# A fused attention and MLP kernel: outputs of 15 attention chunks computed with channels on partitions and turned to rows by DMA, and three moves in the order of the side work

## The reference

```
state = alpha[t, :, None] * state + k[t] (outer) v[t]
y[t]  = q[t] @ state
```

## Time and profile before

| | |
|---|---|
| median of 3 runs | 753.81 us (753.63 to 753.96) |
| the profiled execution | 753.43 us, span in the profile 751.9 us |
| PE busy | 741.3 us, 99% of the span |
| DVE, ACT, POOL busy | 457.1, 300.3, 60.0 us |
| granted PE clock | full speed in all 40 slices |
| chain that ended last | PE 89%, DVE 5%, DMA 2%, ACT 2% |

### The profile page before, as it was taken

How to read it: one execution, slowest core, us unless ns; L and a number is a source line. 1 busy time by engine, 2 the same in 40 slices (tenths; PEclk the granted TensorE clock), 3 DMA queues, 4 the chain that set the end, 5 groups by cost and what they waited for, 6 DMA issues and landing times.

```text
span 751.9 us, 16930 instructions
## 1 busy us (share of the span) xinstructions
PE 741.3 (99%) x6898; PEld 717.1 (95%) x6898; DVE 457.1 (61%) x1056; ACT 300.3 (40%) x517; POOL 60.0 (8%) x124
## 2 busy tenths in 40 slices
PE   8999999999999999999999999999999999999998
PEld 7889989899999899999999999999999999999998
DVE  7887777957677477774786764247443664243322
ACT  3453232626544364463543344143522434141511
POOL 1100000000000000000005000200021000200000
PEclk9999999999999999999999999999999999999999
DMA  8362214273533536335344421040103101010100
GB/s 246 113 172 82 72 43 135 58 175 82 152 77 78 143 104 115 103 112 153 80 137 132 147 48 52 3 135 32 33 32 120 49 16 47 0 35 28 39 25 32
DMA packets 77809, 64.64 MB, mean 86 GB/s; under 512 B 44788, under 2 KB 72680, under 8 KB 77736
## 3 DMA queue, kind: packets, MB, share of 16 engines
q1 hardware_dynamic: 77736, 63.62, 31.7%
HBM read 43.65 MB, written 13.37 MB: 76 GB/s over the span
## 4 chain that ended last, share of the span: by engine, by line
PE 89%; DVE 5%; DMA 2%; ACT 2%; issue 1%; POOL 0%; DVEq 0%; POOLq 0%; ACTq 0%
PE h L125 14%; PE h L127 12%; PE h L126 12%; PE acc L125 12%; PE acc L127 12%; PE acc L126 12%; PE side_bank L1691 2%; DMA kT_planes<-k_planes 2%; PE side_bank L126 2%; PE side_bank L127 2%; PE side_bank L1704 2%; PE side_bank L125 2%; PE side_bank L1622 1%; PE side_bank L1634 1%; DVE F_inv L1146 1%
## 5 line engine op out<-in xcount | busy, mean ns | idle before, releaser
L194 ACT ACTIVATE hT_high<-h 128x384 fp32r<-128x384 f32 (+1 forms) x204 | 96.1, 471 | 319.6 <-PE h L127 319.4
L199 DVE SCALAR_TENSOR_TENSOR hT_low<-h,hT_high 128x384 fp32r<-128x384 f32 (+1 forms) x204 | 108.3, 531 | 172.3 <-ACT hT_high L194 171.3
L125 PE MATMUL h<-xnT_high,w_high 128*128 128x384 f32 (+1 forms) x612 | 207.0, 338 | 0.9 <-DVE w_low L258 0.9
L127 PE MATMUL h<-xnT_high,w_low 128*128 128x384 f32 (+1 forms) x612 | 199.3, 326 | 0.0
L126 PE MATMUL h<-xnT_low,w_high 128*128 128x384 f32 (+1 forms) x612 | 199.2, 325 | 0.0
L125 PE MATMUL acc<-w_high,hT_high 128*128 128x384 f32 x576 | 193.6, 336 | 0.5 <-DVE hT_low L199 0.5
L127 PE MATMUL acc<-w_high,hT_low 128*128 128x384 f32 x576 | 192.8, 335 | 0.0
L126 PE MATMUL acc<-w_low,hT_high 128*128 128x384 f32 x576 | 192.5, 334 | 0.0
L125 PEld LDWEIGHTS h<-xnT_high,w_high 128*128 128x128 f32 x612 | 115.1, 188 | 5.0 <-DVE w_low L258 1.0
L126 PEld LDWEIGHTS h<-xnT_low,w_high 128*128 128x128 f32 x612 | 115.3, 188 | 0.0
L127 PEld LDWEIGHTS h<-xnT_high,w_low 128*128 128x128 f32 x612 | 115.1, 188 | 0.0
(11 more groups left out here) (152 smaller groups left out, 801.0 us busy)
## 6 DMA issues: line engine op xcount, KB each, us to landing
stage<-w_dram SPq DMA_DIRECT2D x24, 384.0 KB, 3.6
x_scratch<-x_unit SPq DMA_DIRECT2D x8, 576.0 KB, 3.6
a_in<-alpha_dram SPq DMA_DIRECT2D x6, 672.0 KB, 4.9
q_in<-q_dram SPq DMA_DIRECT2D x6, 672.0 KB, 6.5
k_in<-k_dram SPq DMA_DIRECT2D x6, 672.0 KB, 8.5
v_in<-v_dram SPq DMA_DIRECT2D x6, 576.0 KB, 3.7
xb<-x_scratch SPq DMA_DIRECT2D x4, 576.0 KB, 4.3
xb<-x_turned SPq DMA_DIRECT2D x4, 576.0 KB, 7.0
```

Of the source, the lines that this page charges most:

```text
L125: pe.matmul(out, wh, xh, start=start, stop=False)
L127: return pe.matmul(out, wl, xh, start=False, stop=stop)
L194: act.activation(self.hT[0][:, j % H_SLOTS, 0:u.cols], self.hps[j % H_BANKS][:, 0:u.cols], ACT.Relu).then_inc(self.h_high, 1)
L199: dve.scalar_tensor_tensor(out=self.hT[1][:, j % H_SLOTS, 0:u.cols], in0=self.hps[j % H_BANKS][:, 0:u.cols], scalar=0.0, in1=self.hT[0][:, ...
```

## The change

The outputs of the 15 REGULAR chunks are computed the other way round. Within the halves `v_in` (48 columns) is stationary and `probs` (64 columns) moving; for the carried part `state` (48 columns) is stationary and `q_mul` (64) moving. The result has channels on partitions; the first half of the tokens goes to `bank[BSC]`, the second to `bank[BY]`, and both parts are summed in place, so `copy_y` and `add_odd` go. ACT splits the result into planes (`split_y`, two ACTIVATEs), SP turns them by DMA (`turn_y`), ACT joins them to rows of x (`join_y`, two ACTIVATEs on 64 partitions each). `u_summed` is now given by the outputs within, behind the increments.

Order: chunk 2's increments and outputs (slots 6, 7) go ahead of `pe_down`. On ACT the range checks move from slots 2 and 3 to 0 and 1, `copy_kT` of chunk 2 from 6 to 5, `split_x` from 8 to 9; `join_x` and the high parts are done for two chunks in slot 10 and for the third in slot 11. On DVE `prepare_q` of the following unit moves from 6 to 7, ahead of the statistics of chunks 0 and 1; chunk 2's statistics come in slot 8 behind `prepare_k`, its normalisation in slot 9. On SP the load of alpha stands first and `load_k` ahead of `turn_k` of chunk 2; `turn_y(ONE[-1], 2)` stands behind `load_rows(0)`.

```diff
         self.next_slot, self.next_k_slot, self.next_q_slot = 6, 8, 10
+        self.ahead = ()
...
         self.rows_slot, self.range_slot = 9, 3
-        self.k_turned = self.x_turned = False
+        self.k_turned = self.x_turned = self.y_turned = False
...
 for u in REGULAR:
-    u.k_turned = u.x_turned = True
+    u.k_turned = u.x_turned = u.y_turned = True
...
     u.x_before, u.units_before = REGULAR[0].base, REGULAR[0].n
-    u.scores, u.increments, u.outputs = (0, 3, 5), (1, 4, 6), (2, 5, 7)
+    u.scores, u.increments, u.outputs, u.ahead = (0, 3, 5), (1, 4, 6), (2, 5, 7), (5, 6, 7)
...
             kT_planes = sb1("kT_planes", [P, 2 * PAIRS, R], U16)
+            y_planes = sb1("y_planes", [R, 2 * PAIRS * P], U16)
+            yT_planes = sb1("yT_planes", [P, 2 * PAIRS, 2 * ODD], U16)
...
         JOINS = {10: (0, 1), 11: (2,)}
+        FRONT, LAST = slice(0, 2 * P), slice(2 * P, UN)
...
             return (bank[BSC], m.hps[1] if u.first() else bank[BY])[two]
+        def yT_bank(i):
+            return (bank[BSC][:, 0:PAIRS * SUB], bank[BY][:, PAIRS * SUB:2 * PAIRS * SUB])[i]
...
                 sp.dma_start(v_in[:, s, :], v[0, :, g, :]).then_inc(first_v[g], 16)
-            def load_qa(u):
-                chunks = slice(u.c0, u.c0 + UT)
+            def load_a(u):
...
                 sp.wait_ge(range_checked, u.n)
-                sp.dma_start(a_in[:, :, :], aT[u.b, :, chunks, :]).then_inc(a_loaded, 16)
+                sp.dma_start(a_in[:, :, :], aT[u.b, :, u.c0:u.c0 + UT, :]).then_inc(a_loaded, 16)
+            def load_q(u):
...
                 sp.wait_ge(q_ready, u.base)
-                sp.dma_start(q_in[:, :, :], qT[u.b, :, chunks, :]).then_inc(q_loaded, 16)
+                sp.dma_start(q_in[:, :, :], qT[u.b, :, u.c0:u.c0 + UT, :]).then_inc(q_loaded, 16)
...
                 sp.dma_start_transpose(kT_planes[:, :, :], k_planes[:, :]).then_inc(kT_turned, 16)
-            def turn_x(u):
-                for c in range(UT):
+            def turn_y(u, c):
+                sp.wait_ge(y_split, u.base + c - FIRST_TURNED + 1)
+                sp.wait_ge(x_ready, u.base + c)
+                sp.dma_start_transpose(yT_planes[:, :, 0:R], y_planes[:, :]).then_inc(y_turned, 16)
+            def turn_x(u, chunks=range(UT)):
+                for c in chunks:
...
                 attending = ONE[u.n - 1]
-                turn_k(attending, 1)
-                load_qa(u)
-                turn_k(attending, 2)
+                load_a(u)
+                if attending in REGULAR:
+                    turn_k(attending, 1)
+                    turn_y(attending, 0)
+                load_q(u)
...
                 load_k(u)
+                if attending in REGULAR:
+                    turn_k(attending, 2)
+                    turn_y(attending, 1)
...
                     turn_rows(*AFTER_K[u.n])
+                if attending in REGULAR:
+                    turn_y(attending, 2)
...
                 load_v(u)
-                if attending.x_turned:
+                if attending in REGULAR:
...
             turn_k(ONE[-1], 1)
+            turn_y(ONE[-1], 0)
...
             turn_k(ONE[-1], 2)
-            turn_rows(2, 1)
+            turn_y(ONE[-1], 1)
...
             load_rows(0)
+            turn_y(ONE[-1], 2)
...
             turn_x(ONE[-1])
+            turn_rows(2, 1)
...
                 wait_apart(x_ready, u.base + u.size)
-                wait_apart(x_odd, u.base + u.size)
+                if not u.y_turned:
+                    wait_apart(x_odd, u.base + u.size)
...
                 inv_std(u, slice(0, u.size))
-            with pool.Fori(1, B) as b:
+            for u in ONE[3:5]:
+                final_rows(u)
+                inv_std(u, slice(0, 2))
+                inv_std(u, slice(2, UT))
+            with pool.Fori(2, B) as b:
...
                     u = Unit(2 * b + half + 1, b, UT * half, UT, half)
+                    u.y_turned = True
...
                                ACT.Copy).then_inc(x_joined, 1)
+            def split_y(u, c):
+                act.wait_ge(y_summed, u.base + c + 1)
+                for i in range(2):
+                    op = act.activation(y_planes[:, :].rearrange("p (w h i t) -> p w h i t", w=2, h=PAIRS, i=2)[:, :, :, i, :],
+                                        yT_bank(i)[0:R, :].bitcast(U16).rearrange("p (h t w) -> p w h t", h=PAIRS, w=2),
+                                        ACT.Copy)
+                op.then_inc(y_split, 1)
+            def join_y(u, c):
+                act.wait_ge(y_turned, 16 * (u.base + c - FIRST_TURNED + 1))
+                if c == 0 or u.slot(c) == 0:
+                    act.wait_ge(stored[u.half(c)], 16 + 16 * u.b)
+                to = x_rows(u)(c).bitcast(U16).rearrange("p (h two d w) -> p w h two d", w=2, two=2, d=D)
+                for i, sub in enumerate(SUBS):
+                    src = yT_planes[sub, :, :].rearrange("p (w h) (two d) -> p w h two d", w=2, two=2)
+                    op = act.activation(to[sub, :, :, :, :], src[:, :, :, ::(1, -1)[i], 0:D], ACT.Copy)
+                op.then_inc(x_ready, 1)
...
                 act.activation(m.xnT[u.par][0][:, k, 0:u.cols], xT_rows(u, k), ACT.Copy, scale=scale).then_inc(xT_high, 1)
+            def high_part(u, k, cols):
+                act.wait_ge(x_joined, u.base - u.x_before + cols.stop // P)
+                act.activation(m.xnT[u.par][0][:, k, cols], xT_over(u)[:, k, cols], ACT.Copy,
...
             def side_regular(u, following, slot):
                 if slot == 0:
                     copy_kT(u, 0)
+                    check_above(u)
+                if slot == 1:
+                    check_below(u)
...
                     split_k(u, 1)
-                    check_above(u)
-                    copy_y(u, 0)
+                    split_y(u, 0)
...
                     copy_kT(u, 1)
-                    check_below(u)
...
                     split_k(u, 2)
+                    join_y(u, 0)
...
                 if slot == 5:
-                    copy_y(u, 1)
+                    split_y(u, 1)
+                    copy_kT(u, 2)
...
                 if slot == 6:
-                    copy_kT(u, 2)
+                    join_y(u, 1)
...
                 if slot == 7:
-                    copy_y(u, 2)
+                    split_y(u, 2)
...
                 if slot == 8:
+                    join_y(u, 2)
+                if slot == 9:
...
                 if slot == 10:
-                    for c in range(UT):
-                        join_x(u, c)
+                    join_x(u, 0)
+                    join_x(u, 1)
+                    for k in range(KD):
+                        high_part(u, k, FRONT)
...
                 if slot == 11:
+                    join_x(u, 2)
...
                     for k in range(KD):
-                        high_xT(u, k, g_col[:, k:k + 1])
+                        high_part(u, k, LAST)
...
             dve.memset(zeros[:, :], 0.0).then_inc(zeros_done, 1)
+            dve.memset(yT_bank(1), 0.0)
...
                                              op0=ALU.mult, op1=ALU.subtract).then_inc(m.xnT_ready, 1)
+            def low_part(u, k, cols):
+                if cols == FRONT:
...
+                else:
+                    dve.wait_ge(xT_high, KD * u.n + k + 1)
+                out_, high = (part[:, k, cols] for part in reversed(m.xnT[u.par]))
+                op = dve.scalar_tensor_tensor(out=out_, in0=xT_over(u)[:, k, cols], scalar=g_col[:, k:k + 1], in1=high,
+                                              op0=ALU.mult, op1=ALU.subtract)
+                if cols == LAST:
+                    op.then_inc(m.xnT_ready, 1)
...
                     dve.wait_ge(x_ready, u.base + i + 1)
-                    dve.wait_ge(x_odd, u.base + i + 1)
+                    if not u.y_turned:
+                        dve.wait_ge(x_odd, u.base + i + 1)
...
         @block.vector
...
             def side_regular(u, following, slot):
...
                 if slot == 2:
                     prepare_q(u, 2)
-                    add_odd(u, 0)
...
                 if slot == 5:
-                    add_odd(u, 1)
...
                 if slot == 6:
+                    next_state(u, 2)
...
                         bound_alpha(following)
-                    next_state(u, 2)
+                if slot == 7:
...
                         prepare_q(following, 0)
-                if slot == 7:
-                    add_odd(u, 2)
-                    final_statistics(u)
+                    final_statistics(u, (0, 1))
...
                 if slot == 8:
-                    normalise(u, x_rows(u), xn_one)
+                    normalise(u, x_rows(u), xn_one, (0, 1))
...
                         prepare_k(following, 0)
+                    final_statistics(u, (2,))
+                if slot == 9:
+                    normalise(u, x_rows(u), xn_one, (2,))
...
                 if slot == 11:
-                    for k in range(KD):
-                        low_xT(u, k, g_col[:, k:k + 1])
```

(55 more changed lines are left out.)

11 lines of the change are left out of this document (8 added, 3 removed).

## The result

The changed kernel took 763.12 us (median of 4 runs, 761.95 to 764.38) against 753.74 us: ratio 1.0124 [1.0107 to 1.0142], 9.4 us slower. The forecast was 759.3 in a range up to 764.5, so the sign and the range held, and the size fell 3.8 us short.

What follows compares the result with a forecast made beforehand. PE, busy 741.3 of 751.9 us, was taken as the bound. New waits of 7.5 + 5.3 + 3.3, less 8.9 and 1.9, gave +5.3 us: 758.7 on the profiled execution, forecast as 759.3, range 747 to 764.5.

Steps and rivals of the forecast that it cites:

- case A: The forecast itself: three new waits outweigh PE's shorter stream, 759.3 us, own range 755.5 to 763; chance 0.62.
- PE's own gain: Side work of 15 chunks: turned outputs within and carried run faster, 0.59 us a chunk, 8.9 us in all.
- old waits that go: PE's existing waits in the hosts, for copied kT and once for the state, should vanish: 1.9 us.
- first wait: Outputs carried of chunk 0, slot 2: check_above ahead of relu(1) delays the state, 7.5 us over five hosts.
- second wait: Unit's end, pe_down(11): longer DVE and ACT chain makes the low part late, 1.3 us in four hosts, 5.3 in all.
- third wait: Increments of chunk 0, slot 1: late split_k delays kT, 0.8 us in four hosts, 3.3 us in all.
- Within 0.54: Turned outputs within take 0.54 us a chunk, saving 0.50, bounds 0.42 to 0.53.
- Carried saves 0.09: Turned outputs carried save 0.09 us a chunk, bounds 0 to 0.10.
- estimate of 11 us more: By the skill's 25 ns rule, within saves 0.13 a chunk, carried loses 0.30, some 11 us worse; prediction sided with the trace.
- The 15 more transposes sit in SP's idle time; each 1.25 us of issue: DMA queue in the hosts: the added transposes fit where SP idles, 1.25 us of issue each, and cost nothing.
- Rival F: kT of chunk 2 lands late behind the load of k, holding slot 6's increments 1.7 us a host: 767; chance 0.04.
- Costs nothing behind the hosts: Last host: turn_y of chunk 2 behind load_rows(0) lands some 1 us late, and pe_up(11) has cover for that.

Runs made afterwards that it cites:

- e1: Changed kernel with check_above put back one slot on ACT, from slot 0 to slot 1, behind relu(1): 758.36 us.
- e7: Kernel before with only the two range checks moved early, to slots 0 and 1 of ACT: 755.87 us.
- e3: Changed kernel with split_k of the following unit moved ahead of split_x of chunk 2 on ACT: 757.70 us.
- e9: Changed kernel with the row copies of batches 1 and 2 taken out of the hosts and issued later in bursts: 768.65 us.
- e5: Changed kernel with check_above behind relu(1), chunk 2's statistics ahead of prepare_k, split_k in slot 9 and one batch 1 row copy later: 758.83 us.
- e11: Changed kernel with check_above behind relu(1), chunk 2's statistics ahead of prepare_k, split_k in slot 9 and row copies issued singly: 750.61 us.

## Why the prediction was right in sign and short in size

The forecast was case A: PE's own stream gets shorter, three waits take more than that back. It named the waits by place and releaser, and all three are there, in the hosts it said. Term by term:

| term of the forecast | forecast | measured |
|---|---|---|
| PE's own gain, 15 chunks | -8.9 | -7.4 |
| old waits that go | -1.9 | -1.0 |
| first wait (outputs carried, chunk 0) | +7.5 | +6.8 |
| second wait (`pe_down(11)`) | +5.3 | +2.9 |
| third wait (kT, slot 1) | +3.3 | +3.1 |
| kT in other slots, n = 5 and 6 | 0 | +2.4 |
| lower clock in n = 5 | 0 | +1.5 |
| pipeline restarts behind waits and the rest | 0 | +0.7 |
| behind and ahead of the hosts | 0 | +1.8 |
| sum, against the span | +5.3 | +10.7 |

- **PE's gain.** "Within 0.54" was 0.56, by records that start every 17.5 ns on average. "Carried saves 0.09" failed: it saves 0.01 to 0.02. The step took the pace to be set by the stationary side, because scores (64 and 64 columns) and carried (64 and 48) ran alike. The turned carried outputs have 48 and 64 and run alike too, so 64 columns on either side go with the slower pace; the increments are the only block with 48 on both. The step also said that the turned form has a bank for each row half. That is so within the halves, but the turned carried outputs write both row halves into either bank, and no run separates the two reasons. The Trainium skill (TensorE: Matmul & The Clock Gate, section "Wait — 56ns, not 53.3ns?") says that starts are never closer than about 25 ns. Counted by records, as the prediction counted, the trace disagrees: the increments' 32 records still take 0.40 us, 12.5 ns each, and the turned 0.56 for 32 is below 25 ns too. Counted by matmuls of the program, two records each, they are 25 and 35 ns apart on average (in pairs closer, as the last section shows), and the rule would not have forbidden the gain; the estimate of 11 us more hung on the count by records.
- **Old waits.** I had worked out 1.9 from the weight loads less the entry gap; by the matmuls' own idle time there were 1.0 to take.
- **First wait.** Right, mechanism and size; e1 takes it away in four hosts and leaves 1.0 in the first, e7 makes it alone.
- **Second wait.** The count holds within 0.4 us at every point. From the end of `pe_up(7)` (212.19) the pair is normalised after 6.8 us (forecast 6.9), `prepare_k` done after 9.4 (9.5), x of chunk 2 normalised after 11.65 (12.0), `split_x` after 12.5 (12.8), relu(11) starts after 16.1 (16.5), the low part is there after 17.1 (17.5), and PE wanted it after 16.4 (16.3). But the wait is a difference of two numbers of 16 to 17 us: 0.4 less in the chain, near half of it POOL's single 1/std, 0.95 from chunk 2's statistics (222.41) to the normalisation (223.36) where I took a pair's 1.1, and 0.1 more cover made 0.7 of 1.3. The mechanism is right; the term was mis-sized by that.
- **Third wait.** Right, and e3 shows it to be worth more than its own line, because the late copy also stood ahead of the check.
- **"The 15 more transposes sit in SP's idle time; each 1.25 us of issue"** is the step that failed outright. A queue's idle time in the profile is not free time for a transpose that PE needs: behind a row copy an issue takes 3 to 5 us, not 1.25. Rival F had this mechanism, a kT that lands behind a load, but in chunk 2's slot and with a chance of 0.04; it came in chunk 1's slot of the one host where the copy falls badly. In chunk 2's slot it came too, but small: 0.57 us in host n = 6, where the transpose behind the load of k landed 6.8 us after its issue and e9, without the copies, has the same; and in the last host of e1 and e5, behind a row copy, 0.98 and 1.51. That n = 5 is the copies is shown by e9. What put alpha's load in between is the change's order, which has `load_a` ahead of `turn_k(attending, 1)` (made possible by the early checks, which free alpha's buffer), where before the transpose came first and was issued at 238.12, alpha's load at 246.82. An early `split_k` of the next unit does not help it (e3 still has this wait, 1.76), nor does the check's place (e1, 1.65).
- **"Costs nothing behind the hosts".** I had looked at `turn_y` behind `load_rows(0)` only. Two row copies stand ahead of the pieces of the table now, and ACT idles 2.94 us for one (L255, 388.22); the wait of 1.1 for `fold_low` comes at 397.90, behind it; that the one makes the other was not followed step by step. That the copies' place is the cause is made likely by e11, where with them spread the tail lasts 379.72; no run moved these two alone.
- **What was not priced at all** is the clock. It fell in the profile of after, in host n = 5. The four executions list mean granted clocks of 0.998 (764.38, 763.28 and 762.95 us) and 1.000 (761.95 us). One fall of 3.4 us in 762 is 0.998, so three of the four had one and the fastest had none. Where it fell in the two that were not profiled is not known: some executions of the kernel before list 0.998 too (754.50 and 754.71 us beside e1, against 753.2 to 754.1 for most at 1.000).

The terms that the forecast had come to +4.4 where it had 5.3, by errors against each other: PE's gain and the old waits 2.4 short, the three waits 3.3 below. Some 6.3 of the 10.7 us are terms that it put at nothing (0 in the table, each rounded): late kT in other slots, the clock, the restarts, and what lies outside the hosts. That the time stayed inside the range is owed in part to luck: the upper bound of 764.5 was not drawn for any of these. The profile's 10.7 against the medians' 9.4 is no further term; the profiled execution is the slowest of the four.

## What to carry to other kernels

A shorter stream on the bound engine makes every hidden chain of the others visible, so a saving must be priced together with the slack of each chain that it shortens the cover of: the form alone was worth 7.4 us of PE's work and gave 4.3 without any other edit. Small work put "where an engine idles" belongs behind, not ahead of, the operation whose result a chain waits for; one move on ACT gave back 4.8 us and another 5.4. And large DRAM-to-DRAM copies on the queue that also issues small urgent transfers have to be issued singly, in places where nothing urgent is next: the same copies cost nothing that shows when spread, 3.4 us in one host (the clock included), and about 6.7 in a burst.
